# Sink transposes of the second attention batch moved one unit earlier, sink products joined to the last product's unit

## What is computed

```python
keep = is_sink | in_window
scores = np.where(keep, scale * q @ k.T, -1e9)
a = softmax(scores); x = a @ v               # heads side by side: x is (2, 768, 512)
h = x.T @ U @ V;  u = x + h.T;  x = u + relu(u @ w_ch1) @ w_ch2          # rank 32, 2048 hidden
h = relu(x.T @ w_tok1) @ w_tok2;  u = x + h.T;  out = u + relu(u @ w_ch1) @ w_ch2   # 256; 1536 hidden
```

## Time and profile before

| what | us |
|---|---|
| median of three runs | 653.14 (652.93 to 653.20) |
| profiled execution, its own time | 653.0 |
| span of its trace, first to last instruction | 651.2 |
| PE busy | 630.7 |
| POOL busy | 367.0 |
| DVE busy | 331.8 |
| ACT busy | 317.2 |

### The profile page before, as it was taken

How to read it: one execution, slowest core, us unless ns; L and a number is a source line. 1 busy time by engine, 2 the same in 40 slices (tenths; PEclk the granted TensorE clock), 3 DMA queues, 4 the chain that set the end, 5 groups by cost and what they waited for, 6 DMA issues and landing times.

```text
span 651.2 us, 10345 instructions
## 1 busy us (share of the span) xinstructions
PE 630.7 (97%) x3532; PEld 565.3 (87%) x3532; DVE 331.8 (51%) x721; ACT 317.2 (49%) x719; POOL 367.0 (56%) x373
## 2 busy tenths in 40 slices
PE   6999999999999999999999999999999999999997
PEld 5888798899889897899999988889998888899986
DVE  7776542333343344377567662186668325676411
ACT  4657555454454453565445444454444455444321
POOL 8545456656555565356756554475756543757262
PEclk9999999999999999999999999999999999999999
DMA  8344254342322515223232333233233342421142
GB/s 180 91 92 118 46 162 115 98 130 81 98 82 82 161 51 161 58 72 112 67 113 82 109 98 102 82 113 99 80 113 98 95 139 91 146 87 44 49 134 93
DMA packets 88276, 65.51 MB, mean 101 GB/s; under 512 B 43008, under 2 KB 72192, under 8 KB 88224
## 3 DMA queue, kind: packets, MB, share of 16 engines
q1 hardware_dynamic: 88224, 64.85, 34.8%
HBM read 61.42 MB, written 3.15 MB: 99 GB/s over the span
## 4 chain that ended last, share of the span: by engine, by line
PE 87%; DVE 4%; ACT 3%; issue 3%; POOL 2%; DMA 0%; ACTq 0%; DVEq 0%; POOLq 0%
PE bank L1356 33%; PE bank L1155 21%; PE bank L1322 10%; PE bank L1185 4%; PE bank L1212 4%; PE bank L1193 3%; PE bank L1286 3%; PE bank L1249 3%; PE bank L1230 2%; PE bank L1170 1%; PE bank L1263 1%; POOL w_lo L753 1%; ACT w_hi L774 1%; PE bank L1348 1%; DVE x_nat L978 1%
## 5 line engine op out<-in xcount | busy, mean ns | idle before, releaser
L753 POOL TENSOR_TENSOR w_lo<-w_raw,w_hi 128x512 fp32r<-128x512 f32 (+1 forms) x158 | 205.6, 1307 | 170.9 <-ACT w_hi L774 170.4
L774 ACT ACTIVATE w_hi<-w_raw 128x512 fp32r<-128x512 f32 (+1 forms) x158 | 96.4, 618 | 60.6 <-PE bank L1356 42.7
L1155 PE MATMUL bank<-b_hi,a_hi 128*128 128x384 f32 x280 | 94.8, 338 | 1.0 <-DVE temps L1065 0.6
L1155 PE MATMUL bank<-b_lo,a_hi 128*128 128x384 f32 x280 | 94.8, 339 | 0.0
L1356 PE MATMUL bank<-w_hi,hid_hi 128*128 128x512 f32 x216 | 87.6, 406 | 0.0
L1356 PE MATMUL bank<-w_hi,hid_lo 128*128 128x512 f32 x216 | 85.1, 394 | 0.0
L1356 PE MATMUL bank<-w_lo,hid_hi 128*128 128x512 f32 x216 | 84.7, 392 | 0.0
L800 ACT ACTIVATE probs<-masked,neg_max 128x264 f32<-128x264 f32 x96 | 49.5, 516 | 68.3 <-DVE neg_max L953 67.8
L1356 PE MATMUL bank<-w_hi,y_hid 128*128 128x512 f32 x216 | 71.1, 394 | 0.2
L953 DVE CUSTOM_DVE_ANT_0 masked<-bank,masks 128x264 f32<-128x264 f32 x96 | 41.2, 430 | 39.5 <-PE bank L1185 35.6
L898 DVE SCALAR_TENSOR_TENSOR hid_lo<-bank,hid_hi 128x384 fp32r<-128x384 f32 x32 | 17.8, 558 | 77.6 <-ACT hid_hi L762 77.6
(11 more groups left out here) (137 smaller groups left out, 1405.8 us busy)
## 6 DMA issues: line engine op xcount, KB each, us to landing
w_raw<-in_moe_w_ch_dram SPq DMA_DIRECT2D x144, 256.0 KB, 2.7
w_raw<-in_moe_w_ch_dram SPq DMA_DIRECT2D x20, 512.0 KB, 3.4
q_nat<-in_q_dram SPq DMA_DIRECT2D x12, 256.0 KB, 3.0
k_nat<-in_k_dram SPq DMA_DIRECT2D x12, 256.0 KB, 3.5
v_nat<-in_v_dram SPq DMA_DIRECT2D x12, 256.0 KB, 3.3
out_dram<-o_stage SPq DMA_DIRECT2D x12, 256.0 KB, 3.4
w_raw<-in_moe_w_tok_dram SPq DMA_DIRECT2D x6, 256.0 KB, 2.7
w_raw<-in_moe_w_tok_dram SPq DMA_DIRECT2D x8, 192.0 KB, 2.3
```

Of the source, the lines that this page charges most:

```text
L753: nc.gpsimd.tensor_tensor(w_lo[:, split % NW, 0:n], w_raw[:, split % NR, 0:n], w_hi[:, split % NW, 0:n].bitcast(f32), ALU.subtract) \
L774: nc.scalar.activation(w_hi[:, split % NW, 0:n], w_raw[:, split % NR, 0:n], ACT.Copy) \
L1155: last = mm(bank[:, 0:HALF], w[at % 2][:, a, k, :], u[:, b_part, k, :], start=(first and n == 0), stop=(n == 5), skip_group_check=True)
```

## The change

Four edits, all on the second batch. The transposes of the sink columns (`sinksT`) are placed at the lag of the transposes, two units behind the tile's last scores, and no longer three. The sink product (`sinkpv`) is no longer a unit of its own; it stands in the unit of the tile's last `pv`, right behind it. Every 16th matmul step took two units before; now each takes one. And one empty unit is put between the attention and `preparation(1, 1)`.

```diff
-            if lo <= u - LAG_V < hi and (u - LAG_V) % H == H - 1:
-                now.append(("sinksT", (u - LAG_V) // H))
+            sinks_after = u - (LAG_T if b else LAG_V)
+            if lo <= sinks_after < hi and sinks_after % H == H - 1:
+                now.append(("sinksT", sinks_after // H))
...
-            elif b == 0:
+            else:
                 pv = pv + late + sinkpv
             now += scores + pv + probsT
...
             units.append(now)
-            if b and sinkpv:
-                units.append(sinkpv)
...
-    waiting = attention(1) + preparation(1, 1)
+    waiting = attention(1) + [[]] + preparation(1, 1)
...
-    n = 0
     for s in mixer(1, 0):
         plan.append(s)
         if s[0] in ("mm1", "mm2", "up") and waiting and not (s[0] == "mm2" and ends(s)):
-            n += 1
             plan += waiting.pop(0)
-            if n % 16 == 0:
-                plan += waiting.pop(0)
```

## The result

The changed kernel takes 654.95 us (median of 8 runs, 654.49 to 657.37), where the kernel before takes 653.14 (8 runs, 652.93 to 654.14). The ratio is 1.0034, with a 95% interval of 1.0024 to 1.0043. So it is slower, by 1.8 us. The forecast was 653.9, in a range from 652.6 to 655.6.

What follows compares the result with a forecast made beforehand. PE's stream of matmuls (busy 97% of the span) was taken as the bound, so only waits and seams could move. The terms -3.2 - 2.6 - 1.3 + 7.0 + 0.9 = +0.8 us on 653.14 gave 653.9, range 652.6 to 655.6.

Steps and rivals of the forecast that it cites:

- The old sink units: Old places of the sink transposes: their extra time, mostly behind `mm1` steps with `hid_lo`, goes; -3.2 us.
- the pairs: Three places with two units behind one matmul step: 8.2 us becomes 5.6 as single units; -2.6 us.
- The wait of `down`: Before `down`: waiting goes, as `x_nat` precedes the additions and two matmul steps lie between; -1.3 us.
- The sink product: Moved into the `pv` unit: same 0.23 us as alone, so 0; bound ±0.5 us over six tiles.
- `kT` behind the sink transpose: Tiles 6 to 9: `kT` waits for the shared bank, starting 1.74 us behind the sink transpose; +7.0 us.
- Tiles 10 and 11: Sink transposes in their new places there: 0.3 us extra for tile 10, 0.6 for tile 11; +0.9 us.
- The additions of tile 10: On DVE, now right before the next masked minimum: they just fit, cost 0; bounds 0 and 2.9 us.
- rival B: Behind tile 10's sink product: additions hold back the masked minimum; slower, 654.7 us, or 655.7 with a third; chance 0.22.
- Rival C: Tiles 6 to 9: the bank wait is 1.04 us, not 1.74; 2.8 less, 651.1 us, faster; chance 0.05.
- rival D: In the `kT` unit: ACT's copy comes sooner, four times 0.25 us goes; 652.9 us; chance 0.12.
- the sign that was named as less likely: Whole kernel: slower, chance 0.34, against 0.59 for the same and 0.07 for faster.

Runs made afterwards that it cites:

- the last experiment: Changed kernel with second-batch sink transposes three units behind the scores, more empty units, and two matmul steps taking two units each: 652.34 us.
- the first four experiments: Changed kernel with one edit each: three empty units, 654.38 us; first edit undone, 651.17; `kT` one unit later, 652.51; sink subtraction ahead of `hid_lo`, 653.38.

## Why the prediction was right, and where not

- **The old sink units, -3.2, and the pairs, -2.6:** right. In after no unit waits for the masked minimum, and the last experiment prices two of the three pairs by themselves; the third (2.30 us in before) and the old sink units have no experiment of their own.
- **The wait of `down`, -1.3:** right. There is no idle time in front of it.
- **The sink product, 0:** a little low. The units with it take 1.17 to 1.19 us where 0.89 + 0.23 = 1.12 was assumed, 0.06 for each, 0.3 in all. That lies within the stated bound.
- **`kT` behind the sink transpose, +7.0:** right, to the hundredth. Each starts 1.74 us behind. The experiments show the mechanism from both sides: with other work between (lag three, `kT` later) the waits go or shrink, and with `hid_lo` out of the chain each is 0.43 shorter.
- **Tiles 10 and 11, +0.9:** right. Their units take 1.21 and 1.22 us.
- **The additions of tile 10, 0:** right. PE does not wait for a masked minimum or a `probs_T` copy there, so rival B did not come. The additions start 2.7 us into the unit and take 2.6, as assumed, and the copy ends at 6.6, just ahead of PE's 6.8. One of the four again met a `w_lo` of POOL: the second took 1.38 us (229.21) beside a `w_lo` that started at 228.92, the other three 0.41 to 0.43. The margin of 0.2 us held, but a second such meeting would have used it up.
- **What failed:** the prediction priced the empty unit and the lost places only at `down`, and said that nothing is late next. The steps behind it moved too. `tsplit`, on which ACT waits 2.24 us for DVE, came two matmul steps earlier, in front of the last `w_hi` copies and `hid_hi`, and the last `mm2` step paid 0.9 us. The prediction's own rule, to name what is queued behind a waiting instruction, was used for `kT` and not here. With 0.8 + 0.9 + 0.3 the sum is +2.0, and +1.8 was measured. The range had room for it because of rival B, which has another cause; so far it was luck that the time fell inside.
- Rival C (a wait of 1.04 us) and rival D (the copy of `kT` sooner) fall: `kT` started at 1.74, and its unit behind it took the same 1.6 us as before.

So the sign that was named as less likely came out. The sum stood at +0.8 us, below the 1.3 that a measurement tells from none, and one missed term of 0.9 lifted it above.

## What to carry to other kernels

When transposes or other products share one bank, the price of a step is the chain that frees the bank, counted from what each engine has in its queue at that moment, less the work that stands before the next user of the bank. So put the step behind a stretch that leaves the draining engines free, and something between it and the next user; its lag alone says nothing. And when the number of slots in a hand-written plan changes, everything that follows moves against its surroundings: look at each instruction in the moved part that waits, and at what is queued behind it.

## What the runs showed of the hardware

In the profiled execution of after the granted clock fell behind the wait of `kT` at tile 9. PE had idled for 1.47 us up to 192.60 and had then been busy again at full clock. In the view by stretches (us, busy time of PE, PEld, DVE, ACT and POOL, granted clock, share and rate of DMA):

```profile
191.00:192.00 1.00, 0.13 (x2) 0.00 (x0) 0.42 (x1) 0.75 (x3) 0.04 (x1) 1.00 0.06 9
192.00:193.00 1.00, 0.40 (x5) 0.43 (x5) 0.85 (x3) 0.00 (x0) 0.01 (x1) 1.00 0.90 215
...
195.00:196.00 1.00, 1.00 (x4) 0.71 (x3) 0.19 (x1) 0.50 (x1) 0.42 (x1) 0.50 0.00 0
196.00:197.00 1.00, 1.00 (x4) 0.80 (x3) 0.50 (x1) 0.00 (x0) 0.86 (x1) 0.50 0.00 0
```

0.50 is the lower of the two levels, 1.2 GHz. The `mm2` step there took 3.73 us and not 2.15, so the fall cost 1.6 us. Within the same run the clock was also at 0.50 from 75 to 78 us. That fall began within the wait for `x_nat` at the end of the first attention (0.85 us idle in front of 75.26), in a part that the change leaves alone. The kernel before has runs with a lower clock as well: 7 of the 27 runs of it beside the first four experiments show a mean clock of 0.997 and times of 654.3 to 654.8 us, the others 652.9 to 654.2. None of these was profiled, so where the clock fell in them is not shown. A mean clock as low as 0.994 is in one run alone, the profiled one of after (657.37 us). Whether the waits of `kT` make such a fall likelier stays open; eight runs are too few, and no experiment aimed at it.
